# Attention's first round finished before the next scores, and its first loads in a hand-written order on one queue

## What is computed

```python
def _attn_ref(q, k, v) -> np.ndarray:          # q, k, v: (4, 8, 768, 64)
    B, H, S, D = q.shape
    gamma = 1.0 - 2.0 ** (-5.0 - np.arange(H, dtype=np.float32))
    scale = 1.0 / np.sqrt(D)
    state = np.zeros((B, H, D, D), dtype=np.float32)
    y = np.zeros_like(q)
    for t in range(S):
        state = gamma[None, :, None, None] * state + np.einsum('bhd,bhe->bhde', k[:, :, t], v[:, :, t])
        y[:, :, t] = scale * np.einsum('bhd,bhde->bhe', q[:, :, t], state)
    return y.astype(np.float32)

def reference(**kwargs):
    ...
    attn_out = _attn_ref(**attn_kwargs)
    B, H, S, D = attn_out.shape
    x = np.ascontiguousarray(attn_out.transpose(0, 2, 1, 3)).reshape(B * S, H * D)
    x = _moe_ref(x=x, **moe_kwargs)            # (x @ w_a * (x @ w_b)) @ w_out
    return _moe2_ref(x=x, **moe2_kwargs)       # each row through the one expert of its gate
```

## Time and profile before

| | us |
|---|---|
| device time, median of three runs | 1030.89 (1030.52 to 1032.0) |
| the profiled execution's own time | 1030.35 |
| its span, first to last instruction | 1028.5 |
| PE busy in the span | 1012.5 (98%) |

### The profile page before, as it was taken

One profiled execution on the slowest core, in us unless ns is written; L12 is line 12 of the kernel. 1 busy time (PEld: TensorE's weight loads), 2 busy tenths in 40 slices (PEclk: granted clock), 3 DMA queues, 4 the chain that ended last, 5 costly groups with the idle time before them and its releaser, 6 DMA issues.

```text
span 1028.5 us, 17407 instructions
## 1 busy us (share of the span) xinstructions
PE 1012.5 (98%) x5761; PEld 841.5 (82%) x5762; DVE 553.4 (54%) x1211; ACT 283.7 (28%) x490; POOL 120.2 (12%) x108
## 2 busy tenths in 40 slices
PE   6999999999999999999999999999999999999998
PEld 5898888888888888888888878888888888888886
DVE  3455342487567747773877323466554635354642
ACT  2554331221212122112211212131533424333431
POOL 4870000000000000000000000001211111211211
PEclk9999999999999999999999999999999999999999
DMA  9998700511061114103310312021754334254311
GB/s 365 368 322 264 198 1 1 144 58 46 1 158 47 41 32 133 52 31 82 93 52 21 83 41 81 2 62 41 288 178 142 134 109 164 88 175 156 114 42 37
DMA packets 53865, 114.37 MB, mean 111 GB/s; under 512 B 8749, under 2 KB 23405, under 8 KB 53296
## 3 DMA queue, kind: packets, MB, share of 16 engines
q1 hardware_dynamic: 48752, 98.95, 30.4%
q0 software_dynamic: 4480, 13.91, 4.0%
q10 hardware_dynamic: 576, 0.79, 0.2%
HBM read 96.81 MB, written 17.61 MB: 111 GB/s over the span
## 4 chain that ended last, share of the span: by engine, by line
PE 98%; DMA 1%; issue 0%; SPq 0%; DVE 0%; POOL 0%; ACT 0%; DVEq 0%; POOLq 0%
PE bank L1078 38%; PE bank L1109 19%; PE bank L1442 15%; PE bank L1466 14%; PE bank L1450 2%; PE bank L606 2%; PE bank L559 2%; PE bank L671 1%; DMA rows<-in_steps 1%; PE bank L593 1%; PE bank L573 1%; PE bank L1165 0%; PE bank L985 0%; PE bank L852 0%; PE bank L1151 0%
## 5 line engine op out<-in xcount | busy, mean ns | idle before, releaser
L1078 PE MATMUL bank<-x_hi,wab_hi 128*128 128x512 f32 x576 | 224.5, 390 | 0.0
L1078 PE MATMUL bank<-x_hi,wab_lo 128*128 128x512 f32 x576 | 224.1, 389 | 0.0
L1078 PE MATMUL bank<-x_lo,wab_hi 128*128 128x512 f32 x576 | 224.1, 389 | 0.0
L1007 DVE SCALAR_TENSOR_TENSOR products<-y_sb,gate_row 128x512 f32<-128x512 f32 x256 | 176.9, 691 | 23.7 <-DMA gate_row<-xT_dram 16.4
L1442 PE MATMUL bank<-w,xe 128*128 (+1 forms) x648 | 158.9, 399 | 0.5 <-DVE xe L695 0.5
L1442 PEld LDWEIGHTS bank<-w,xe 128*128 128x128 f32 x648 | 119.4, 188 | 28.1 <-issue 1.8
L1019 DVE TENSOR_TENSOR g_sb<-bank,b_sb 128x512 f32<-128x512 f32 x72 | 49.7, 690 | 168.2 <-PE bank L1078 168.2
L1078 PEld LDWEIGHTS bank<-x_hi,wab_hi 128*128 128x128 f32 x576 | 108.2, 188 | 22.8 <-issue 0.3
L1078 PEld LDWEIGHTS bank<-x_lo,wab_hi 128*128 128x128 f32 x576 | 108.2, 188 | 22.4
L1078 PEld LDWEIGHTS bank<-x_hi,wab_lo 128*128 128x128 f32 x576 | 108.1, 188 | 22.4
L1109 PE MATMUL bank<-wo_hi,g_hi 128*128 128x512 f32 x288 | 113.4, 394 | 0.0
(11 more groups left out here) (172 smaller groups left out, 1067.7 us busy)
## 6 DMA issues: line engine op xcount, KB each, us to landing
raw<-in_w SPq DMA_DIRECT2D x64, 512.0 KB, 6.1
gate_row<-xT_dram SPq DMA_DIRECT2D x64, 256.0 KB, 3.2
rows<-in_steps SPq DMA_DIRECT2D x20, 768.0 KB, 7.9
rows<-in_steps SPq DMA_DIRECT2D x24, 256.0 KB, 7.2
wab_raw<-in_weights SPq DMA_DIRECT2D x24, 256.0 KB, 8.5
x_rows<-y_sb SPq DMA_DIRECT2D x6, 1024.0 KB, 9.0
xT_dram<-x_all SPq DMA_DIRECT2D x4, 1024.0 KB, 11.9
x_raw<-xT_dram SPq DMA_DIRECT2D x16, 256.0 KB, 8.2
```

The source lines that it names most:

```text
L1007: nc.vector.scalar_tensor_tensor(products, y_sb[:, t], 1.0, gate_row[e % GATE_SLOTS], ALU.mult, ALU.mult, accum_out=L3[:, t, e:e + 1]).the ...
L1078: ins = nc.tensor.matmul(to, wab(w, f, j), x[s][:, k, :], start=(k == 0 and m == 0), stop=(k == KD - 1 and m == 2))
```

## The change

Two things change.

On SP's queue the first round's loads are taken apart: first q and k transposed of step 0 (512 KB, with a semaphore of its own, `first_in[0]`), the two masks, q and k transposed of step 1 (`first_in[1]`), then k and v of step 0, k and v of step 1, and the q table. ACT keeps only `kdec_t`. Rounds 1 and 2 follow as before. GpSimd's first q product waits for `first_in[1]` as well, since `qk_in` now stands for k alone in the first round.

On TensorE, `cross` and `within` of round 0 come ahead of the loop, right behind `kv` of round 0, and so ahead of `scores` and `kv` of round 1. Inside the loop they are left out in its first pass by an If on `b > 0`, for j = 0 only.

```diff
@@ -278,6 +278,7 @@
     v_in = [sem(f"v_in{c}") for c in range(CH)]
+    first_in = [sem(f"first_in{i}") for i in range(ROUND)]
     wab_in = [sem(f"wab_in{q}") for q in range(HALVES)]
@@ -387,7 +388,19 @@
-        for r in range(RB):
+        def load_first(i):
+            sp.dma_start(rows[:, i, 0:2], steps_in[i][:, 0:2]).then_inc(first_in[i], 16)
+
+        load_first(0)
+        for o in range(2):
+            sp.dma_start(mask_t[o].rearrange("p a t -> p (a t)"),
+                         const_in[:, C_MASK + o * PAIRS * P:C_MASK + (o + 1) * PAIRS * P]).then_inc(mask_in[o], 16)
+        load_first(1)
+        for i in range(ROUND):
+            sp.dma_start(rows[:, i, 2], steps_in[i][:, 2]).then_inc(qk_in[i], 16)
+            load_v(0, i)
+        sp.dma_start(qdec_t, const_in[:, C_QDEC:C_MASK]).then_inc(qdec_in, 16)
+        for r in range(1, RB):
             for i in range(ROUND):
                 load_qk(r, i)
                 load_v(r, i)
@@ -455,6 +468,7 @@
                 if (b, c) == (0, 1):
                     pool.wait_ge(qdec_in, 16)
+                    pool.wait_ge(first_in[1], 16)
@@ -483,11 +497,7 @@
-        for o in range(2):
-            act.dma_start(mask_t[o].rearrange("p a t -> p (a t)"),
-                          const_in[:, C_MASK + o * PAIRS * P:C_MASK + (o + 1) * PAIRS * P]).then_inc(mask_in[o], 16)
         act.dma_start(kdec_t, const_in[:, C_KDEC:C_QDEC]).then_inc(kdec_in, 16)
-        act.dma_start(qdec_t, const_in[:, C_QDEC:C_MASK]).then_inc(qdec_in, 16)
@@ -549,8 +559,10 @@
         def scores(b, j, first=False):
             for i, c in chunks(j):
-                pe.wait_ge(qk_in[c], 16 * b + 16 * (j // RB + 1))
-                if not first:
+                if first:
+                    pe.wait_ge(first_in[i], 16)
+                else:
+                    pe.wait_ge(qk_in[c], 16 * b + 16 * (j // RB + 1))
                     pe.wait_ge(probs_done, CH * b + ROUND * j - ROUND + i + 1)
@@ -609,6 +621,8 @@
         scores(0, 0, True)
         kv(0, 0, True)
+        cross(0, 0)
+        within(0, 0)
         with pe.Fori(0, B) as b:
@@ -620,8 +634,13 @@
                     with pe.If(b > B - 2):
                         first_up()
-                cross(b, j)
-                within(b, j)
+                if j == 0:
+                    with pe.If(b > 0):
+                        cross(b, j)
+                        within(b, j)
+                else:
+                    cross(b, j)
+                    within(b, j)
```

## The result

The changed kernel takes 1033.94 us (median of 12 runs, 1033.17 to 1035.21) against 1031.04 of the kernel before, measured beside it: a ratio of 1.0026, 95% interval 1.0017 to 1.0035. I had forecast no change, 1029.5 to 1032.2. The profiled execution took 1034.16 us with a span of 1032.3, 3.8 longer than before. (Of a later kernel, e8, one execution took 2071.26 us; its ratio leaves it out.)

The account below looks back on a forecast made before the run. Round 3's v landing at 30.0 us was taken to bound the kernel. Moved work -2.5, waits for steps 4 and 5 +1.6, `kv` gap -0.6, longer v wait +1.5 summed to 0: profiled 1030.35, median 1030.9, range 1029.5 to 1032.2.

Parts of the forecast that it names:

- The landing of round 3's v fixes the end: At `kv` of round 3: v landing at 30.0 us sets the moment from which TensorE never idles again.
- The landing stays at 30.0: Round 3's v on the DMA queue: the change moves its landing by 0, with 0.5 us on both sides.
- The line of 2.7 us per MB: DMA queue: landing times fitted against MB asked for, starting at 3.65 us, used to place the changed first-round loads.
- rival (c): Start of the queue: split loads and one queue move the landing over 0.5 but under 2 us; chance 0.12, half each side.
- `cross` and `within` of round 0 take 0.6 and 1.9 us: First round on TensorE: moved forward, they start at 12.4 us and end at 14.9 instead of 20.74.
- the limit of the cover: Round 0's `within` may end as late as 19.1 us without cost; expected 14.9, so 4 us late costs nothing.
- `kv` of round 1 still ends at 18.3, and 1.5 us are left at round 3: TensorE, rounds 1 to 3: 2.5 us won at 18.3; ahead by 1.5 us when round 2's `within` ends at 25.4.
- Requests moved within a full queue cost nothing: SP's loads: asking for round 3's v 0.7 us earlier brings nothing; a first round 4 us late costs nothing.
- Rival (b): `kv`, `cross`, `within` at round 3: clock falls in the 2.6 us gap, +3.4 us, median 1034.3; chance 0.05.

Follow-up runs that it names:

- e8: Changed kernel with SP asking for v of round 3 ahead of q and k of round 4; 1032.28 us, ratio 1.0010.
- e1: Kernel before with only TensorE's order changed (`cross` and `within` of round 0 moved forward), old loads; 1032.87 us, ratio 1.0013.
- e2: Changed kernel without the moved `cross` and `within`, so only the loads differ from the kernel before; 1032.63 us, ratio 1.0016.
- e6: Kernel before with SP asking for v of round 3 ahead of q and k of round 4; 1030.78 us, ratio 0.9999.
- e13: e6 with 32 semaphore increments ahead of the first scores, moving all later TensorE code by 32 instructions; 1031.02 us, ratio 1.0000.
- e4: Kernel before with the first round's steps loaded whole, masks and q table between them on SP's one queue, old order; 1031.68 us, ratio 1.0007.
- e16: e15 without the 5 unneeded matmuls between scores and `kv` of round 3; 1031.33 us, ratio 1.0005.
- e15: e1 with unneeded matmuls filling the first round's pauses, plus 5 between scores and `kv` of round 3; 1031.61 us, ratio 1.0009.
- e14: Changed kernel with unneeded matmuls in each first-round pause to keep TensorE busy; 1032.64 us, ratio 1.0017.
- e17: e16 with v of round 3 asked for ahead of q and k of round 4; 1031.06 us, ratio 1.0000.
- e5: e1 with 8 unneeded matmuls put between scores and `kv` of round 3 to fill the pause; 1032.80 us, ratio 1.0012.
- e7: e1 with SP asking for v of round 3 ahead of q and k of round 4; 1031.64 us, ratio 1.0007.
- e12: Meant as e6 with 64 register moves, which are not in the trace, so the same program as e6; 1031.08 us, ratio 1.0006.
- e3: e2 with masks and q table back on ACT's queue: loads split, two queues, old order; 1032.74 us, ratio 1.0015.

## Why the prediction was wrong, step by step

- *The landing of round 3's v fixes the end.* Right for the kernels where TensorE comes in time: e1 goes on within 0.1 us of the first v (30.1), e2 within 0.1 us of the second (32.3). It is right for the changed kernel too, with the second v at 34.1. Incomplete: code arrives at nearly the same moment (e6, e13), which no row I read shows.
- *"The landing stays at 30.0."* Wrong, and the largest failed step. It was 32.2 and 34.1 for the two steps in the changed kernel, and 31.6 and 32.3 with the loads alone (e2), whose `kv` of round 3 ended 1.8 us late. I gave ±0.5 for it. The line of 2.7 us per MB was fitted to whole steps on one queue with ACT's beside it and applied to another mix. By it round 1's q and k stay at 13.1 and 15.6; they came at 15.5 and 18.1, the sign that I had named for rival (c). That rival had the mechanism, but with a size "over 0.5 us but under 2" at 0.12, half of it as a gain, on no row that would show a loaded start with one queue. The row that could have warned me was the 333 GB/s of the first 15 us: I put the whole shortfall down to latency.
- *`cross` and `within` of round 0 take 0.6 and 1.9 us.* Mis-sized: 1.13 and 3.61. I had the low level of the first round in front of me, used it for `scores` and `kv` of round 0 and took the full-level length from the earlier trace rows for two operations that I moved into that same stretch. `within` ended at 20.2, past the 19.1 that I had called the limit of the cover.
- *`kv` of round 1 still ends at 18.3, and 1.5 us are left at round 3.* Even with the old loads and the full level from 14.0 on (e1) it ended at 20.0, VectorE's probs added a wait of 0.67 us that the sum lacks, and 0.4 us were left.
- *Requests moved within a full queue cost nothing.* True only as long as the queue is full. `kv` of round 1 ended 5.6 us late, q and k of round 4 were asked for at 23.8, and the rate fell to 245 GB/s. I had checked this cover for one cause of lateness, not for slow loads and low clock at once. e8 got 1.4 us back by one swap.
- *Rival (b), the clock falls in the longer gap.* The right kind of loss, at 0.05 far too low. In the changed kernel's own profile it is a late rise rather than a fall, so that its 1034.3 us lie near the measured 1033.94 is chance. In e1, e4 and e16 it is the fall, after pauses of 1.77, 2.30 and 2.04 us, where I had argued from 1.14 and 1.17 us that paused work is safe. Pauses of 1.63, 1.73 and 1.76 us (e6, e13, e15) brought no fall. It costs less than I put (e1: 1.5 us on 4.3, not 3.4), because the level came back inside `within`. The Trainium skill (TensorE: Matmul & The Clock Gate, HAM oscillation) says that a wait for data puts TensorE back to the lower clock and the work behind it starts cold; here the trace agrees, 1.00 before and 0.50 from 31.1 us in e1.

Added up by medians, each less the kernel before beside it: the changed kernel loses 2.9 us, the loads alone 1.8 (e2), and the order on top of them about 1.1 (changed kernel less e14). That this last part is the clock's is argued more than shown, since e14 changes the clock and the times of the requests together. e8's 1.4 us can't be added to it: low clock, late `kv` of round 1, late requests and late v are one chain, and the two kernels break it at different places. Of the 2.5 us of work that the order puts into idle time, 0.4 reached round 3 in e1 and went into the wait for v. With v early and the clock up, 1.15 us reached the end of `kv` of round 3 in e17's profiled execution, and part of that went into a wait for code.

## What to carry to other kernels

When work is moved into an idle stretch, price it with the durations of that stretch: if TensorE is at its lower level there, the moved work is slower, and if the move leaves longer pauses behind, so may be what follows. A cover is only as good as the queue that makes it full: ask how late a buffer may come free before the queue runs dry, with all the change's delays added. And where the profile names no releaser for a pause, look for a second wait that ends at the same time, and for one that is no data at all: moving the code by some instructions tells.

## What the hardware showed that I had not expected

- TensorE's code waits for instructions in the loop's first pass: blocks of 16 KB that took 0.9 to 1.1 us each beside full data queues, and pauses of 0.3 to 2 us with no semaphore, ending 1.3 to 1.7 us after the block. The pause moved with the code (e13). The Trainium skill (Runtime: NRT & Kernel Launch, Instruction fetch mechanics) says that the cost of a block boundary is mostly hidden and that a taken branch may stall; the first half doesn't hold for these pauses. Those shown here stand inside a row of matmuls, with no branch beside them; whether the branches of the loop play a part I didn't try.
- The same first loads (2.9 MB in all) run at 294 GB/s over the first 10 us as whole steps on two queues, at 265 when split, 256 on one queue and 246 both ways, with the DMA share at 0.78 to 0.80 in all.
- The moment at which TensorE gets its full level differs by 4 us between executions with the same loads and the same first-round order: 14.0 in one and 18.0 and 18.1 in two others (e1, e5, e7). With the old order and whole steps it was 13.5 to 14.4 (the kernel before, e4, e6, e12, e13), with the split loads 18.1 to 21.9 (e8, e3, the changed kernel, e2). What sets it isn't shown.
